# Loading two experts' weights and the gates one piece per attention head instead of all in the first head

## What is computed

```
q_pool = q.reshape(B, H, S // factor, factor, D).mean(axis=3)      # B 2, H 8, S 1152, D 64, factor 2
scores = scale * np.matmul(q_pool, k.transpose(0, 1, 3, 2))
attn = softmax(scores); x = np.matmul(attn, v)                      # to 1152 tokens x 512
logits = x @ w_gate; e_idx = argmax(logits); gate_w = its softmax
eom = sigmoid(x @ w_output_gate)
for e in range(8):
    h = np.maximum(x[mask] @ w1[e], 0.0)                            # w1 8x512x1024
    out[mask] = gate_w * eom[e] * (h @ w2[e])                       # w2 8x1024x512
h = out @ w_in; y = (h * tanh(softplus(h))) @ w_out                 # d_ff 2048
```

## Time and profile before

| | us |
|---|---|
| median of 3 runs | 677.72 (677.46 to 678.32) |
| the profiled execution | 679.0 |
| its span in the trace | 677.3 |
| PE busy | 664.0 (98%) |
| DVE, ACT, POOL busy | 504.9, 409.7, 92.0 |
| granted TensorE clock, mean | 0.998 |

### The profile page before, as it was taken

How to read it: one execution, slowest core, us unless ns; L and a number is a source line. 1 busy time by engine, 2 the same in 40 slices (tenths; PEclk the granted TensorE clock), 3 DMA queues, 4 the chain that set the end, 5 groups by cost and what they waited for, 6 DMA issues and landing times.

```text
span 677.3 us, 14740 instructions
## 1 busy us (share of the span) xinstructions
PE 664.0 (98%) x5135; PEld 591.9 (87%) x5135; DVE 504.9 (75%) x1180; ACT 409.7 (60%) x839; POOL 92.0 (14%) x136
## 2 busy tenths in 40 slices
PE   8999999999999999999999999999999999999996
PEld 6889898988898999579999999899998988899995
DVE  5777677777777776676666676676999998887873
ACT  5767576666666666554656475666676655445542
POOL 7705040505041200220000000000000000101001
PEclk9999999999999999999999999999999999999999
DMA  8888869797977600469990752041200000001001
GB/s 182 186 274 211 249 146 259 181 261 176 264 172 204 150 2 9 174 244 395 398 367 16 279 199 83 15 156 54 86 1 1 1 0 1 32 16 47 1 0 47
DMA packets 95351, 93.83 MB, mean 139 GB/s; under 512 B 41920, under 2 KB 70976, under 8 KB 94784
## 3 DMA queue, kind: packets, MB, share of 16 engines
q1 hardware_dynamic: 91536, 84.39, 42.8%
q10 hardware_dynamic: 2320, 4.00, 1.9%
q0 software_dynamic: 1440, 4.72, 1.8%
HBM read 59.80 MB, written 16.78 MB: 113 GB/s over the span
## 4 chain that ended last, share of the span: by engine, by line
PE 81%; SPq 6%; DVE 5%; POOL 2%; issue 2%; ACT 2%; DMA 0%; ACTq 0%; DVEq 0%; POOLq 0%
PE score_banks L1161 14%; PE score_banks L1191 11%; PE score_banks L1176 10%; PE pvT L902 9%; PE turn L922 9%; PE score_banks L1213 4%; PE pvT L1213 4%; PE turn L1213 4%; PE score_banks L873 4%; PE score_banks L874 4%; SPq L560 2%; PE score_banks L879 1%; PE turn L823 1%; PE turn L1139 1%; PE turn L1148 1%
## 5 line engine op out<-in xcount | busy, mean ns | idle before, releaser
L1261 ACT ACTIVATE prob<-score_banks,nmax 128x1152 f32<-128x1152 f32 x72 | 88.0, 1222 | 51.8 <-DVE nmax L1527 51.8
L922 PE MATMUL turn<-ident,prob 128*128 128x128 f32 x648 | 102.4, 279 | 0.5 <-DVE probT L1583 0.5
L1161 PEld LDWEIGHTS score_banks<-xsT,w_slot 128*128 128x128 f32 x832 | 94.6, 192 | 2.2 <-issue 1.4
L1161 PE MATMUL score_banks<-xsT,w_slot 128*128 x832 | 95.2, 276 | 0.7 <-ACT xsT L1395 0.7
L1266 ACT ACTIVATE probT<-turn 128x384 f32<-128x384 f32 x144 | 69.9, 487 | 36.7 <-PE turn L922 36.7
L922 PEld LDWEIGHTS turn<-ident,prob 128*128 128x128 f32 x648 | 75.1, 141 | 15.0 <-issue 11.0
L902 PE MATMUL pvT<-probT,v_sb 128*64 128x128 f32 (+1 forms) x1404 | 85.9, 269 | 0.0
L902 PEld LDWEIGHTS pvT<-probT,v_sb 128*64 128x64 f32 x1404 | 69.5, 137 | 11.9 <-issue 11.9
L873 PE MATMUL score_banks<-kT,qT 128*128 128x384 f32 x192 | 70.7, 368 | 1.7 <-DMA kT<-k_lo 1.2
L1748 DVE TENSOR_TENSOR w_lo<-w_slot,w_hi 128x512 fp32r<-128x512 f32 x104 | 69.2, 689 | 3.3 <-ACT w_hi L1421 3.2
L1517 DVE TENSOR_REDUCE nmax_part<-score_banks 128x1 f32<-128x768 f32 x72 | 68.3, 949 | 2.0 <-PE score_banks L874 1.8
(11 more groups left out here) (261 smaller groups left out, 1332.8 us busy)
## 6 DMA issues: line engine op xcount, KB each, us to landing
w_slot<-moe_w SPq DMA_DIRECT2D x16, 2048.0 KB, 15.4
slots_dram<-zeros SPq DMA_DIRECT2D x8, 1472.0 KB, 11.6
raw_k<-k SPq DMA_DIRECT2D x16, 288.0 KB, 6.0
v_sb<-v SPq DMA_DIRECT2D x16, 288.0 KB, 4.6
w_in_sb<-moe_w_in SPq DMA_DIRECT2D x2, 2048.0 KB, 7.7
w_out_sb<-moe_w_out SPq DMA_DIRECT2D x2, 2048.0 KB, 9.3
raw_q<-q SPq DMA_DIRECT2D x14, 256.0 KB, 3.4
qT<-q_hi SPq DMA_DIRECT2D x28, 128.0 KB, 2.4
```

Source lines behind the costliest of these rows:

```text
L922: last = pe.transpose(bank[:, j * P:(j + 1) * P], prob[:, s % 2, c * KC + j * P:c * KC + (j + 1) * P], ident[:, :])
L1161: last = pe.matmul(h1_bank[f % 4][:, 0:P], w1_e[:, d, f * P:(f + 1) * P], xsT[:, d, bass.ds((t % XS_RING) * P, P)], start=(d == 0), stop=( ...
L1261: act.activation(prob[:, s % 2, :].rearrange("p (c n) -> p c n", c=NC), scores[s % 2][:, :, 0:KC], ACT.Exp, bias=nmax[:, s:s + 1], accum_o ...
```

## The change

Expert 0's two weight matrices and the gates no longer follow `restack(1)`. In the loop body for h = 1 `w1` of expert 0 takes the place of `w1` of expert 1. For h = 2, 3 and 4 one piece each is put between `restack(h + 1)` and the two pieces of zeros: `w2` of expert 0, `w1` of expert 1, the gates. The same bytes are loaded to the same places, with the same semaphores.

```
+            def load_gates():
+                for n, w in enumerate((w_gate, w_ogate)):
+                    sp.dma_start(w_both[:, :, n * NE:(n + 1) * NE], w.rearrange("(t p) e -> p t e", p=P)
+                                 ).then_inc(wg_landed, 16)
...
             load_kq(2)
             load_v(1, 1)
             restack(1)
-            for n, w in enumerate((w_gate, w_ogate)):
-                sp.dma_start(w_both[:, :, n * NE:(n + 1) * NE], w.rearrange("(t p) e -> p t e", p=P)
-                             ).then_inc(wg_landed, 16)
-            load_expert(0, 0)
...
                 restack(h + 1)
                 if h == 1:
-                    load_w1(1, 1)
+                    load_w1(0, 0)
                     sp.wait_ge(zeros_ready, 1)
                 else:
+                    if h == 2:
+                        load_w2(0, 0)
+                    elif h == 3:
+                        load_w1(1, 1)
+                    elif h == 4:
+                        load_gates()
                     for n in range(2 * (h - 2), min(2 * (h - 1), ZERO_PARTS)):
```

## The result

The changed kernel is slower, as forecast, and by more than the sum said:

| | before | after |
|---|---|---|
| median, us | 678.02 (677.46 to 679.63, 4 runs) | 685.4 (682.6 to 687.68, 4 runs) |
| ratio | | 1.0105 (95%: 1.0086 to 1.0125) |
| the profiled execution: time / span | 679.0 / 677.3 | 684.31 / 682.6 |
| mean granted clock of the profiled execution | 0.998 | 0.995 |

What follows compares the result with a forecast made beforehand. TensorE, busy 98% of the span, was taken as the bound, so only its waits count. Head 2's -1.49 us plus 5.54 us of stalls gave +4.1 us on 677.72: 681.8 us, range 677.0 to 686.3.

Steps and rivals of the forecast that it cites:

- the sum: Whole kernel: head 2's gain plus stalls at heads 4 and 5, -1.49 + 5.54 = +4.1 us; chance 0.70.
- The wait at head 2 goes: Head 2's split keys: restack(2) starts at 55.84, keys land at 69.4, wanted at 71.28; wait goes wholly.
- -1.49 us: Head 2: time gained by removing TensorE's key wait, read from the rhythm as 34.04 - 32.55 us.
- A load of 2048 KB costs 5.4 us of queue: Bodies for h = 2 and 3: 2.10 MB at 388 GB/s takes 5.4 us; 5.1 and 6.2 kept as ends.
- Head 4's keys late by 1.57 us: Restack for head 4: keys land at 139.29, with 12.87 us from restack start to landing, but are wanted at 137.72.
- the short end: Shortest restack length taken, behind a pause: 11.74 us to the landing, 11.40 us to SP's release.
- Head 5's 3.97 us more: Restack for head 5: keys land at 175.81, wanted at 170.27; 5.54 us late in all, 3.97 us more.
- The gates cost nothing at head 6: Body for h = 4: gates hold SP 1.2 us; keys 5.31 us late, under the 5.54 already lost, so 0.
- Absorbed: Bodies for h = 2 and 3: each load costs under 2.6 us and is given back; 676.2 us, chance 0.12.
- the 5.1 us that are free once: Body for h = 2: lateness that costs nothing once, 1.44 + 1.14 + 2.5 us; per head only 2.6 given back.
- Just paid: Loads near 5 us, short restack: about 1.5 us lost, at head 5 alone; 677.7 us, chance 0.13.
- No gain at head 2: Head 2's wait is the restack's own pace, not its late start; 683.3 us, chance 0.05.

Runs made afterwards that it cites:

- the single ones: Four kernels: changed kernel's late loads behind the last restack, except one 2048 KB load: w2 or w1, h = 2 (1.0026, 1.0017); w1 or w2, h = 3 (0.9992, 0.9994).
- the extra turns: Changed kernel, TensorE's passes of two heads written out, plus 12 and 20 identity turns ahead of the waits for head 4's and 5's keys: 685.32 us, ratio 1.01.
- its comparison: Changed kernel with TensorE's four passes of two heads written out one behind the other instead of first pass, loop of two and last pass: 686.12 us, ratio 1.0118.

## Why the prediction came out as it did

**The wait at head 2 goes: right; -1.49 us: too large.** The wait is gone in every trace of a kernel without weights in the first head. But the size was read from one execution. There it was 1.22 us of idle, in the second profile 0.35. The prediction saw that the profiled execution lay 1.3 us above the median and took it as a constant offset; part of it was this wait. Taking all of it away, with everything behind the last restack, gave 0.16% (1.1 us) by the ratio and 0.8 us by the medians.

The late start of `restack(2)` was also only one part of the wait's cause. SP's timeline in the trace of before, at the copy that TensorE waited for:

```profile
69.17 1.70 SPq L585 DMA_DIRECT2D kT<-k_lo  x1
```

and the DMA view from 69 to 70 us:

```profile
q8 instruction: 1, 0.02, 9.0%
```

The copy landed 3.29 us after its issue, with an instruction transfer at 69.0. With the usual 2.2 us it would have landed at 71.4, and TensorE wanted it at 71.28: of the 1.22 us of idle 1.1 are this one copy. In the second trace of before it took 2.82 us. The late start used up the cover, and this delay then fell on TensorE.

**A load of 2048 KB costs 5.4 us of queue: right.** The stretch grew by 5.8 us with `w2` (over 18.53) and by 4.8 with `w1` (over 18.29); by the single ones, 5.4 and 5.1 for h = 2, 4.7 for h = 3. Without a load the stretch for h = 2 itself lay between 18.5 and 19.1 us, so the two weights are not told apart. A third piece of zeros did the same (5.6).

**Head 4's keys late by 1.57 us: right in kind, small.** 2.15 and 2.2 us in the two profiles. The restack took 12.87 us to the landing (125.43 to 138.30), the value chosen, and the rest is the stretch. But the reason given for that value was misread. The row it came from (89.90) also had a pause ahead of it, 2.55 us from the values' end at 87.35. It was longer than the short end, 11.74, by the copy at 92.38, which held SP for 1.71 us behind an instruction transfer. The length fitted head 4 because its restack again had such a transfer, and a first copy held for 1.26 us.

**Head 5's 3.97 us more: the time was near, the make-up not.** 2.5 us of rhythm in the execution without a fall, and 4.63 with one, of which 1.7 is the clock. The term was oversized for the queue. In that execution the stretch with `w1` was 22.63 us and not 23.93, and head 4 had already taken 0.6 us more of the lateness than forecast. And the term left the clock out. The queue's part of both heads is 4.7 us in that execution and was forecast at 5.54.

**The gates cost nothing at head 6: right** in both profiles, and with more room than the 0.23 us of the sum. The stretch with the gates was 18.87 and 18.93 us, about 0.5 more than without (18.41) and not 1.2. In the kernel after head 6's last batch 0 copy was issued at 203.58 and TensorE came to its keys at 208.29, 4.7 us later, where 2.2 would have done. With the extra turns there was a short wait there, in PE's timeline of that run:

```profile
207.66 0.45 PE L880 MATMUL score_banks<-kT,qT 128*128 128x384 f32 x1 [0.29 <-DMA kT<-k_lo]
```

There the last batch 0 copy, issued at 204.16, took 3.45 us to land instead of 2.2, with an instruction transfer at 204.6; it is no sign that the sum's narrow margin was right.

**The step that failed is the one that was not there: the clock.** The forecast of +4.1 us is what an execution without a fall does: 681.85 was measured, 681.8 forecast, though by luck in part: by two errors of 0.7 to 0.8 us that cancel, stalls forecast too long and a gain forecast too large. The median is 3.6 us higher. Over the runs of the kernel after and of its comparison the time goes with the mean clock: 682.6 us at 0.996, 684.15 to 685.24 at 0.995, 686.5 to 688.0 at 0.993. With `w2` alone for h = 2 the same: 679.26 to 680.69 at 0.997 to 0.999, 681.51 to 683.27 at 0.994 to 0.996 (one run of 681.85 at 0.997). That is about two microseconds for a fall; the profiled fall took 1.7 us of work here and 3.4 in the run with a third piece of zeros, where it lasted from 139.9 to 146.7 us. Two of its windows are

```profile
142.00:144.00 2.00, 2.00 (x13) 1.67 (x13) 0.80 (x3) 0.49 (x1) 0.00 (x0) 0.50 0.96 206
144.00:146.00 2.00, 2.00 (x20) 1.67 (x17) 0.20 (x1) 0.00 (x0) 0.00 (x0) 0.50 1.08 321
```

The clock need not be all of it. As an estimate from the mean clocks, the two slowest runs of the kernel after lost (0.998 - 0.993) x 687 = 3.4 us to falls and would have taken 683.1 and 684.3 us without them, 1.3 to 2.5 above the forecast. These runs have no trace, so how their excess divides between clock and waits stays open.

The single idle of 1.22 us in the trace of before, at full clock, was no evidence for waits of 2 to 3 us, and the prediction should have named the fall as a cost without a row and widened for it.

**The rivals.** Absorbed: refuted by the waits at heads 4 and 5. A load in the body for h = 3 alone brings no wait either, but not because it is cheap for the queue: its stretch grew by 4.7 us, and the 5.1 us that are free once took it. Just paid: refuted, the stalls were 6.8 us in the one profile, with the clock's fall, and 4.7 in the other. No gain at head 2: refuted by the rhythm of 32.55 us there.

## What to carry to other kernels

A queue that serves both bulk loads and the short copies a busy engine waits for has a room per round, to be read as the sum of its pauses there plus the time between landing and use; a load larger than that room is harmless only if the next rounds can give it back. A length read from one trace holds whatever fell into it, here a copy delayed by more than a microsecond, so it should be read in several rounds, and the cause of the longest one looked for. Bulk that is needed late belongs behind the last round with a deadline, or in the place of other bulk. And a new wait of two or three microseconds of TensorE should be priced with the clock's fall behind it.

## What was not expected of the hardware

- TensorE's clock fell to one half with waits of 1.89, 2.47, 2.58 and 2.79 us (with `w2` alone at 140.1, half a microsecond before the wait ended), and not with waits of 1.22, 1.59, 1.78, 1.85, 2.24 and 2.68 us; so the length of the wait alone does not decide it. Why the one at 2.68 left it at 1.00 and the one at 1.89 did not is open.
- The same kernel's chain through SP's queue ended at different times in different executions: the kernel before waited 1.22 or 0.35 us at head 2, and its runs spread from 677.1 to 681.7 us, where the kernel with nothing to wait for stayed within 0.5 us.
- SP's issue of a copy, 0.60 us as a rule, was held for 2.40 us where the values' small pieces and the weights were still in transfer, with an instruction transfer at 56.9.
- Behind instruction transfers of 16 KB, the 58 copies' issues took 0.95 to 2.05 us instead of 0.60, and a key copy issued or in flight then landed in 2.8 to 3.7 us instead of 2.2 (2.82 and 3.29 in the two traces of before, 3.74 with only the gates moved, 3.13 and 3.45 in the two with TensorE's program written out). That each such hold has its transfer is shown in all 14 traces; that the transfer makes it is not tested.
